# Moving the transposed-activation buffer x2T by eight words (32 bytes) in SBUF

## The reference

```python
# 1 attention, q, k, v of shape (4, 8, 768, 64): causal window of 128 keys plus 4 sink keys
scores = q @ k.T / 8 ; softmax over the kept keys ; attn = a @ v
x = attn.transpose(0, 2, 1, 3).reshape(3072, 512)
# 2 mixture of experts: 8 experts, each token goes to the best one
logits = x @ w_gate + modality_bias[modality_id]      # (3072, 8)
out[mask] = gate_w[mask, None] * (np.maximum(x[mask] @ w1[e], 0.0) @ w2[e])   # F = 1024
# 3 dense feed-forward
h = x @ w_in                                          # (3072, 512) @ (512, 2048)
g = h * (1.0 / (1.0 + np.exp(-1.702 * h)))
return g @ w_out                                      # (3072, 2048) @ (2048, 512)
```

## The kernel before

| buffer | start | start mod 64 |
|---|---|---|
| ident | 16,512 | 0 |
| k_lo (slot s, query tile i) | 43,040 + 3,168 s + 528 max(i-1, 0) | 32, 48, 0, 16 |
| w_hi, w_lo | 18,080 and 50,848 | 32 |
| win_hi, win_lo | 83,616 and 116,384 | 32 |
| g32, gT_hi, gT_lo | 149,152, 153,248 and 161,440 | 32 |
| x2T | 180,128 | 32 |
| o_out | 212,928 | 0 |

## Time and profile before

### The profile page before, as it was taken

One profiled execution on the slowest core, in us unless ns is written; L12 is line 12 of the kernel. 1 busy time (PEld: TensorE's weight loads), 2 busy tenths in 40 slices (PEclk: granted clock), 3 DMA queues, 4 the chain that ended last, 5 costly groups with the idle time before them and its releaser, 6 DMA issues.

```text
span 1115.8 us, 18740 instructions
## 1 busy us (share of the span) xinstructions
PE 1100.6 (99%) x5952; PEld 942.0 (84%) x5953; DVE 424.8 (38%) x1089; ACT 377.8 (34%) x781; POOL 326.1 (29%) x441
## 2 busy tenths in 40 slices
PE   9999999999999999999999999999999999999998
PEld 9999999987888888888878888888888888888887
DVE  5566666685122233212264223223223222322222
ACT  3666666643222233222344222222222222222222
POOL 8888888645641212212121001001001001000100
PEclk9999999999999999999999999999999999999999
DMA  9999999237111133211142001001001000000101
GB/s 222 217 258 236 239 229 229 72 124 264 38 47 47 47 108 127 75 47 38 38 147 89 20 1 56 19 0 47 27 1 47 19 9 28 9 0 1 38 1 38
DMA packets 57392, 92.04 MB, mean 82 GB/s; under 512 B 7936, under 2 KB 32768, under 8 KB 57344
## 3 DMA queue, kind: packets, MB, share of 16 engines
q1 hardware_dynamic: 51584, 72.56, 24.3%
q0 software_dynamic: 5760, 18.89, 4.8%
HBM read 72.02 MB, written 19.41 MB: 82 GB/s over the span
## 4 chain that ended last, share of the span: by engine, by line
PE 91%; DVE 4%; ACT 2%; issue 2%; DMA 1%; ACTq 0%; DVEq 0%; POOL 0%; SPq 0%; POOLq 0%
PE psum L981 8%; PE psum L982 8%; PE psum L983 8%; PE psum L972 8%; PE psum L974 8%; PE psum L973 8%; PE psum L789 5%; PE psum L938 4%; PE psum L940 4%; PE psum L913 4%; PE psum L915 4%; PE psum L914 4%; PE psum L939 4%; PE psum L764 2%; PE psum L925 2%
## 5 line engine op out<-in xcount | busy, mean ns | idle before, releaser
L1643 DVE TENSOR_TENSOR g<-psum,g 128x512 f32<-128x512 f32 x96 | 66.3, 691 | 295.0 <-ACT g L1176 295.0
L1176 ACT ACTIVATE g<-psum 128x512 f32<-128x512 f32 x96 | 57.4, 598 | 307.5 <-PE psum L974 304.0
L972 PE MATMUL psum<-x2T,win_hi 128*128 (+1 forms) x384 | 149.6, 390 | 2.3 <-DVE g L1643 2.3
L981 PE MATMUL psum<-w_hi,gT_hi 128*128 128x512 f32 x384 | 151.3, 394 | 0.0
L983 PE MATMUL psum<-w_hi,gT_lo 128*128 128x512 f32 x384 | 149.6, 390 | 0.0
L982 PE MATMUL psum<-w_lo,gT_hi 128*128 128x512 f32 x384 | 149.6, 389 | 0.0
L974 PE MATMUL psum<-x2T,win_lo 128*128 (+1 forms) x384 | 149.5, 389 | 0.0
L973 PE MATMUL psum<-x2T,win_hi 128*128 (+1 forms) x384 | 149.4, 389 | 0.0
L721 POOL DMA_INDIRECT out<-o_out,out_rows x20 | 21.5, 1075 | 412.6 <-ACT o_out L1189 408.1
L789 PE MATMUL psum<-v_sb,pT 128*128 128x73 f32 x704 | 105.9, 269 | 2.4 <-DVE pT L1397 1.2
L1385 DVE CUSTOM_DVE_ANT_0 s_msk<-psum,mask_sb 128x260 f32<-128x260 f32 (+1 forms) x192 | 75.0, 403 | 70.6 <-PE psum L753 38.2
(11 more groups left out here) (229 smaller groups left out, 1988.5 us busy)
## 6 DMA issues: line engine op xcount, KB each, us to landing
qk_raw<-qkT SPq DMA_DIRECT2D x64, 384.0 KB, 8.2
stage<-w SPq DMA_DIRECT2D x12, 1024.0 KB, 6.8
x<-y_rows SPq DMA_DIRECT2D x24, 256.5 KB, 2.7
vT_sb<-vT SPq DMA_DIRECT2D x16, 384.0 KB, 9.4
v_sb<-vP SPq DMA_DIRECT2D x16, 384.0 KB
x_rows<-x_sb SPq DMA_DIRECT2D x16, 384.0 KB, 5.7
win_raw<-w_in SPq DMA_DIRECT2D x16, 256.0 KB, 10.3
stage<-w_out SPq DMA_DIRECT2D x4, 1024.0 KB, 6.6
```

Of the source, the lines that this page charges most:

```text
L972: pe.matmul(bank, wh, hi, start=(c == 0), stop=False)
L981: pe.matmul(psum[:, OB[t], :], gh, hi, start=(f == 0), stop=False)
L1643: dve.tensor_tensor(g32[:, f % 2, :], psum[:, FB[f % 2], :], g32[:, f % 2, :], ALU.mult)\
```

## The change

`x2T` starts eight words later: the 8 words between it and `o_out` are gone, and its start is byte 180,160 where it was 180,128. Its start mod 64 becomes 0. No instruction, wait, transfer or size is changed, and no other buffer moves.

```diff
@@ -269,8 +269,8 @@
-        assert top[0] <= ZS - X2W - 8
-        x2T = place("x2T", [P, 2 * X2W], F32R, at=ZS - X2W - 8)
+        assert top[0] <= ZS - X2W
+        x2T = place("x2T", [P, 2 * X2W], F32R, at=ZS - X2W)
         o_out = place("o_out", [P, GT, DM], at=ZS + X2W)
```

## The result

The changed kernel takes 1128.53 us (median of six runs, 1128.02 to 1129.54) against 1118.09 us for the kernel before in the same comparison. The ratio is 1.0093, with a 95% interval of 1.0083 to 1.0104: 10.4 us slower. The forecast was no change, with a range up to 1121.0 us; slower had 0.09.

What follows compares the result with a forecast made beforehand. The prediction took the feed-forward to be bound by TensorE's matmul stream. Its terms (x2T matmuls, ACT and DVE writes, vanished gap) summed to 0 against the profiled 1117.76 us; from the median it forecast 1118.3 us, range 1115.5 to 1121.0 us.

Steps and rivals of the forecast that it cites:

- What bounds the kernel: Feed-forward: bound by TensorE's stream; 384 matmuls of 0.2267 us make 87.0 of a group's 88.95 us.
- The 1152 matmuls at 0 ns each: Lines 972 to 974, which read x2T as moving operand: the new start changes their distance by nothing, 1152 x 0 = 0.
- near bound: For the x2T matmuls: 1 ns each, from attention-stage durations, 1.2 us either way in all.
- far bound: For the x2T matmuls: the 10 ns resolution of the starts, 11.5 us either way in all.
- the control that I had named: Feed-forward lines 981 to 983, which do not read x2T: they must not move in any case.
- my own sign: If lines 981 to 983 move too, the cause lies in writes to gT or an interplay that no row shows.
- the attention pairs: Attention stage, 260-column matmuls with k_lo at 0 and 32 mod 64: 281 against 282 ns and 287 against 286, so no effect.
- The rival "x2T no longer lies in step": Feed-forward streams at different positions mod 64 make x2T matmuls start some 10 ns late: 11.5 us, 1129.8 us; chance 0.08.
- The rival "faster": The 13.3 ns surplus per feed-forward matmul is partly the offset start: 7.7 us saved, 15.4 if all; chance 0.07.
- The writers: ACT and DVE writes to x2T: term 0, covered by 3.3 us a chunk; as a slower rival, chance 0.01.

Runs made afterwards that it cites:

- e12_odd8: Kernel before with only the odd half of x2T 32 bytes later, where the change has it; 1124.11 us, ratio 1.0047.
- e14: Every ffn_up matmul cut into two of 256 columns, with x2T where the change has it; 1128.41 us, ratio 1.0086.
- e13: Kernel before with every ffn_up matmul cut into two of 256 columns, x2T in its old place; 1135.41 us, ratio 1.0151.
- e9_ident: Kernel before with the identity matrix declared after table, in step with the operands it turns; 1117.64 us, ratio 0.9992.
- e1: The changed kernel with every other matrix operand also moved 32 bytes later, so all at 0 mod 64; 1119.29 us, ratio 1.0009.
- e8: Kernel before with win_lo 32 bytes off and the buffers above it, gT, xsT and hT among them, moved by 128 bytes; 1137.65 us, ratio 1.0162.
- e10: Kernel before with gT_lo alone of the stationary operands 32 bytes off; 1125.32 us, ratio 1.0056.
- e7: Kernel before with every use of x2T starting 4 bytes (1 word) later; 1134.12 us, ratio 1.0131.
- e3_win_0: Kernel before with win_hi and win_lo moved by 32 bytes and the buffers above, xsT, hT, g32 and gT, by 64; 1137.47 us, ratio 1.0173.
- e11_odd64: Kernel before with the odd half of x2T 256 bytes later, o_out as well, even half unmoved; 1118.55 us, ratio 0.9994.

## Why the prediction was wrong

**What bounds the kernel** was right: the time of the stage is the number of matmuls times their distance, and 1.75 us a group times six is the whole loss.

**The 1152 matmuls at 0 ns each** is the step that failed. The term measured 10.5 us, which is 9.1 ns for each of the 1152, nine times the near bound of 1 ns that I had taken. The far bound of 10 ns (11.5 us) held it, but I had left it outside my range. Of the 9.1 ns some 7 are in the matmuls with `x2T` themselves (0.234 against 0.227 us); the rest falls on `ffn_down` behind them, whose own operands are in step. e12_odd8 shows it right behind the odd half:

```profile
702.07 0.40 PE L981 MATMUL psum<-w_hi,gT_hi 128*128 128x512 f32 x1
702.31 0.39 PE L982 MATMUL psum<-w_lo,gT_hi 128*128 128x512 f32 x1
...
703.69 0.39 PE L982 MATMUL psum<-w_lo,gT_hi 128*128 128x512 f32 x1
...
704.82 0.40 PE L972 MATMUL psum<-x2T,win_hi 128*128 x1
```

Seven distances take 1.62 us, 0.231 each, and only the next five, 1.13 us, are back at 0.226. A stream that was late stays late for seven more matmuls. So the control that I had named, lines 981 to 983, did move. By my own sign the cause then lies in the writes to `gT` or in an interplay between matmuls, and these rows show the second.

**The reason for 0 ns** was the attention pairs. They compared an absolute place, 0 against 32 mod 64. The quantity is the distance between two operands, modulo 256 and not 64, and three of the four matmuls (slots 2, 3 and 0) had a moving and a stationary operand out of step: by the addresses, `k_lo` at 0, 96 and 64 mod 256 against 160 for `q_st`, and 160 too for the part of `probs` that is loaded beside L753. Only slot 1 was in step (160), and its 286 ns against 287 shows no gain. At 256 columns the sign of the effect is the other one (e14 against e13), so a pair of 260 columns could not stand in for 512. I had named that weakness and given it no weight. The rows of the feed-forward itself held a warning: every pair of operands of the 512-column matmuls was in step, so the trace had no sample of what the change makes.

**The rival "x2T no longer lies in step"** was right in that a relative place decides and a matmul starts late. Its period of 64 bytes was wrong, and nothing shows that the writes it also named play a part. Its size, 11.5 us and 1129.8 us against 1128.53 us measured, was in part luck. The 10 ns were read from two rows rounded to 10 ns; to the nanosecond that distance is 233 ns, 6 above 227, which would have given some 7 us. And the matmuls of `ffn_down`, which pay a fourth of the loss, were not in its sum. The late starts that lent it the price stand behind transposes, and e9_ident shows that these are there with all operands in step too. Its chance of 0.08 was the error, and the argument against it was again the attention stage.

**The rival "faster"** fell. The 13.3 ns above the columns stay at 32-byte-aligned and 64-byte-aligned starts alike (e1). **The writers** were harmless, as forecast: 581 and 692 ns.

**The cause** is shown as far as this: in matmuls of 512 columns the distance in SBUF between the moving and the stationary operand decides how far apart they start. That 256 bytes are free and 32, 64, 96 and 128 are not is measured. Of the 32-byte grid 0 is the only free place for `x2T`; the others cost 1.29 to 1.93 us a group. That it is the stationary operand loaded beside the read, the one of the next matmul, rests on where the largest step falls in e8 and e10. The writes of ACT and DVE are an unlikely cause. Between 640 and 1020 us ACT is busy for 94 us and DVE for 108 us of the 380, while every `ffn_up` of the changed kernel takes 2.80 to 2.81 us for its twelve distances, against 2.72 to 2.73 us before. That the two reads meet in the same part of the memory is the simplest reading, and it is not shown. Still open are why one load in three slows a stream nearly as much as three (e10), why one word is worst (e7), and why 256 columns prefer the other place (e14). For the first, the seven late matmuls of e12_odd8 suggest a reading that no run tests: where a load out of step comes every third matmul, the stream never settles.

The Trainium skill says of the weight load ("TensorE: Matmul & The Clock Gate", section Step-by-step: what each phase is for) that the array has two independent SBUF read ports, so that loading the next weights does not steal bandwidth from the running matmul. No run here contradicts it for operands in step, but for operands out of step these runs differ: in e3_win_0 the moving operands stayed where they were and their stationary partners were moved, and the matmuls start 0.233 us apart and no longer 0.227. The measurement decides that the two are not independent in time; whether it is read bandwidth that is lost, no run shows.

## What to carry to other kernels

Treat the placement of matmul operands as a parameter where TensorE's stream is the bound: compare the start addresses of the moving and the stationary operand modulo 256 bytes, keep them equal for 512 columns, and measure it anew for another width or type, since only this fp32 form was run. A row of the trace can stand in for an edit only if it shares the quantity that the edit changes; here that was a distance between two buffers, and I had read an address. And PE at 99% busy hides a loss of this kind: count matmuls per microsecond, or take the period of a loop from the chain.

## What the runs showed that I had not expected

Shifting a buffer by 4 bytes cost 1.3% of the kernel (e7_skip1), and shifting one half of it by 256 bytes nothing (e11_odd64). A matmul of 512 columns costs 13.3 ns above its columns at best here, and one of 256 columns 12.9 ns in step (119.6 - 106.7) and 10.0 ns out of step. Two matmuls of 256 columns in step take 239 ns against 227 for one of 512, so halving all of `ffn_up` cost only 1.5% (e13_half_in), where one of my two cases, the weight load of 188 ns setting the distance, had some 19%.
